# The first MLP's rank product one matmul group earlier, and the ranks behind the gating of that step

## The reference

```
attn = softmax(mask(q k^T / 8)) v            # 4 x 8 heads, 576 rows, windowed masks
h = x @ w_in;  g = h * cos(h);  y = g @ w_out                # first MLP: 2304 x 512, 2048 wide
noisy = y @ w_gate + log1p(exp(y @ w_noise)) * noise         # 8 experts
top2 of noisy; weights = softmax of the two
out[t] = sum over both choices of weight * relu(y[t] @ w1[e]) @ w2[e]   # 1024 wide
```

## Time and profile before

| | us |
|---|---|
| median of 3 runs (lowest to highest) | 1034.51 (1033.92 to 1035.71) |
| the profiled execution's own time | 1036.34 |
| its span | 1034.5 |
| TensorE busy in the span | 997.1 (96%) |
| TensorE weight loads | 877.4 (85%) |
| VectorE busy | 584.7 (57%) |
| ScalarE busy | 446.6 (43%) |
| POOL busy | 355.4 (34%) |

### The profile page before, as it was taken

How to read it: one execution, slowest core, us unless ns; L and a number is a source line. 1 busy time by engine, 2 the same in 40 slices (tenths; PEclk the granted TensorE clock), 3 DMA queues, 4 the chain that set the end, 5 groups by cost and what they waited for, 6 DMA issues and landing times. The chain is left out here.

```text
span 1034.5 us, 17745 instructions
## 1 busy us (share of the span) xinstructions
PE 997.1 (96%) x6176; PEld 877.4 (85%) x6176; DVE 584.7 (57%) x1190; ACT 446.6 (43%) x1087; POOL 355.4 (34%) x348
## 2 busy tenths in 40 slices
PE   6989899999999999999999999999999999999994
PEld 5777789888889889889887779999998889899993
DVE  4777867667576586576675744444243444444221
ACT  5878755454454544534547333333132323333110
POOL 2555687322222222222232355142341514241321
PEclk9999999999999999999999999999999999999998
DMA  8787337000000000005006154434342525333220
GB/s 171 172 183 158 76 111 266 32 2 1 30 1 0 30 1 30 1 0 183 12 11 225 59 177 133 150 99 137 139 163 106 192 109 174 126 109 108 78 69 29
DMA packets 101383, 99.63 MB, mean 96 GB/s; under 512 B 72835, under 2 KB 73315, under 8 KB 101312
## 3 DMA queue, kind: packets, MB, share of 16 engines
q1 hardware_dynamic: 89696, 67.16, 21.9%
q0 software_dynamic: 10000, 31.15, 9.6%
q10 hardware_dynamic: 1616, 0.39, 0.2%
HBM read 80.61 MB, written 20.07 MB: 97 GB/s over the span
## 5 line engine op out<-in xcount | busy, mean ns | idle before, releaser
L1740 POOL TENSOR_TENSOR g_lo<-gate,g_hi 128x384 fp32r<-128x384 f32 x95 | 98.0, 1032 | 283.4 <-ACT g_hi L1044 283.3
L1104 ACT ACTIVATE uh_hi<-ps 128x306 fp32r<-128x306 f32 (+1 forms) x112 | 47.8, 426 | 280.1 <-PE ps L155 275.0
L154 PE MATMUL ps<-ux_lo,w_hi 128*128 128x306 f32 (+1 forms) x448 | 136.5, 305 | 0.0
L155 PE MATMUL ps<-ux_hi,w_hi 128*128 128x306 f32 (+1 forms) x448 | 136.0, 304 | 0.0
L153 PE MATMUL ps<-x_hi,w_lo 128*128 128x384 f32 x384 | 134.1, 349 | 1.8 <-DVE gate L1258 1.1
L153 PE MATMUL ps<-ux_hi,w_lo 128*128 128x306 f32 (+1 forms) x448 | 135.8, 303 | 0.0
L1479 DVE SCALAR_TENSOR_TENSOR uh_lo<-ps,uh_hi 128x306 fp32r<-128x306 f32 (+1 forms) x112 | 53.3, 476 | 137.4 <-ACT uh_hi L1104 133.8
L155 PE MATMUL ps<-x_hi,w_hi 128*128 128x384 f32 x384 | 129.2, 337 | 0.0
L154 PE MATMUL ps<-x_lo,w_hi 128*128 128x384 f32 x384 | 129.2, 336 | 0.0
L153 PE MATMUL ps<-w_hi,g_lo 128*128 128x512 f32 x288 | 114.1, 396 | 0.0
L155 PE MATMUL ps<-w_hi,g_hi 128*128 128x512 f32 x288 | 114.0, 396 | 0.0
(11 more groups left out here) (225 smaller groups left out, 2002.8 us busy)
## 6 DMA issues: line engine op xcount, KB each, us to landing
xT<-in_w SPq DMA_DIRECT2D x32, 1024.0 KB, 9.1
out<-table SPq DMA_DIRECT2D x18, 256.0 KB, 3.8
y_rows<-y_sb SPq DMA_DIRECT2D x6, 768.0 KB, 3.5
y_sb<-in_w_out SPq DMA_DIRECT2D x16, 256.0 KB, 3.1
q_raw<-in_q SPq DMA_DIRECT2D x40, 96.0 KB, 2.7
v_raw<-in_v SPq DMA_DIRECT2D x28, 128.0 KB, 2.6
k_raw<-in_k SPq DMA_DIRECT2D x37, 96.0 KB, 2.9
w_raw<-in_w_in SPq DMA_DIRECT2D x4, 512.0 KB, 5.2
```

What stands on the lines that cost most here:

```text
L154: nc.tensor.matmul(psum, s_hi, m_lo, start=False, stop=False)
L155: return nc.tensor.matmul(psum, s_hi, m_hi, start=False, stop=stop)
L1104: nc.scalar.activation(u_h[0][:, f, piece_at[piece]], psH[:, f % 2, 0:PIECE[piece]], ACT.Relu).then_inc(u_hhi, 1)
L1740: nc.gpsimd.tensor_tensor(g2[1][:, f % 2, :], gate[:, f % 2, :], g2[0][:, f % 2, :], ALU.subtract).then_inc(glo_done, 1)
```

## The change

On TensorE `rank(i - 1)` (and in tile 5 `count()`) is issued at the end of step 8, behind `second(i, 6)` and ahead of `first(i, 9)`. On VectorE `route(.., 8)` is issued behind `gates(i, 8)`, ahead of `whole(i, 9)`. The one-hot rows and columns of slot products 0 and 1 stay in step 9 between `fine` and `gates`; `to_table` stays where it is, and so do `route(.., 5)` and `route(.., 6)` in step 7. No instruction is added or taken out.

```diff
@@ TensorE, tile(i)
                     first(i, f)
                     if start and f == 3:
                         second(i, 0)
-                    if not start and f == 9:
-                        rank(i - 1)
-                        if last:
-                            count()
                     if last and f >= FC - 2:
 ...
                     if last and f == FC - 1:
                         transpose_x(0)
+                    if not start and f == 8:
+                        rank(i - 1)
+                        if last:
+                            count()
                     if not start:
                         route(i - 1, f)
@@ VectorE, tile(i)
                     if not first and f == 9:
-                        route(i - 1, link, 8)
                         hots(i - 1, 0)
                     if not first and 9 <= f <= 13:
                         hots(i - 1, f - 8)
 ...
                     if not first and f == 7:
                         route(i - 1, link, 6)
+                    if not first and f == 8:
+                        route(i - 1, link, 8)
```

## The result

The changed kernel took 1039.58 us (median of 5 runs, 1039.11 to 1041.44) against 1034.51 (five runs of the kernel before by then): a ratio of 1.0049, 95% interval 1.0038 to 1.0061. The forecast was 1040.1, range 1038 to 1043.5.

A forecast was written before the change was run, and what follows sets the result against it. TensorE, busy 96% of the span, was taken to bound the kernel. Losses of 4 x 1.08 + 1.29 = 5.6 us on 1034.51 gave 1040.1, range 1038 to 1043.5 (the forecast case's own range 1038.5 to 1041.8).

The forecast's parts named there:

- The rank product: TensorE, end of step 8: it waits for the expert marks, a stall of 1.67 us in each of tiles 1 to 5.
- The terms behind it: TensorE, through first 11: a removed wait returns some 0.46 us, shorter groups 0.13; net loss 1.08 a tile, 1.29 in tile 5.
- The move on VectorE: Ranks, 1.25 us, from step 9 to step 8: costs and gives nothing on TensorE; gates(9) ends at 306.22 again.
- the hold by POOL: VectorE beside POOL's g_lo(8): one rank instruction held some 0.8 us, gates(9) ends at 307.0, still ahead of first 11.
- that rival: TensorE's clock falls after the stalls: at most 1.7 us each, 8.5 more if all five, 1048.6; chance 0.11.
- The rival without a stall: Marks are ready before TensorE reaches the moved rank product, so not slower: 1034.0 to 1034.5; chance 0.06.
- The third: Stall paid, but waits of first 10 and 11 were fixed costs: up to 1.67 us a tile, 1042.9; chance 0.08.
- The profiled execution: Whole kernel under the profiler: 1036.34 us before, forecast 1041.9; the median lies 1.83 lower, giving 1040.1.

The follow-up runs named there:

- the free product: VectorE's ranks behind gates(8), plus two bf16 matmuls on constants at the end of step 8, against the kernel before: 1034.81 us, ratio 1.0002.
- TensorE's half alone: Only the rank product (and count) moved to the end of step 8, VectorE as before, against the kernel before: 1039.98 us, ratio 1.0066.
- VectorE's half alone: Only the ranks on VectorE moved behind gates(8), rank product still in step 9, against the kernel before: 1034.67 us, ratio 1.0002.
- spread one-hots: Kernel before with one-hots of slot products 1 to 5 moved to steps 10 to 13, slot products one step behind: 1032.75 us, ratio 0.9986.
- the marks later: Changed kernel with nine copies of 8 columns ahead of the last marks instruction: 1049.25 us, ratio 1.0140 to the kernel before.

## Why the prediction was right

**The rank product.** The stall was put at 1.67 us a tile and measured 1.66. It is fixed by two times that the trace of before showed: the end of second 6 and the end of the marks. That it is the wait and not the place was argued before and is shown by the free product, and that it is the whole loss by TensorE's half alone.

**The terms behind it.** For tile 2: rank product 0.09 (forecast 0.09), first 9 2.22 (2.22), second 7 2.09 (2.08), first 10 2.08 (2.12), second 8 2.09 (2.08), two slot products 0.19 (0.14), first 11 2.15 (2.17). The loss is 1.07 (1.08). In tile 5 it is 1.23 (1.29): first 9 was 2.17 instead of 2.22 and first 11 2.12 instead of 2.17. Sum 5.49 (5.6). (Tile 1 of the kernel before was not within 0.02 us of the pattern, as the forecast had it: its first 11 took 2.18, that of tile 2 2.22.) The slot products were mis-sized, since I doubled one that follows a group, and the second costs 0.12.

**The move on VectorE** was forecast to change nothing, and VectorE's half alone gave 1.0002. The reason was partly wrong. I let whole, coarse and fine take 2.08 us in any order and bounded the hold by POOL as something added. In fact it is a trade: one of the ranks is held, and `fine(9)`, which was the one beside POOL before, is 0.62 shorter. In tiles 2, 4 and 5 it is the last of the ranks, by 0.70 us (0.87 instead of 0.17), and `gates(9)` began 4.73 us behind `gates(8)`; in tiles 1 and 3 it is the last but one, by 0.85, and they were 4.91 apart. Before, they were 4.88 apart, and the bound had allowed up to 5.7. Tile 3 of the changed kernel, where POOL's subtraction begins at 375.25:

```profile
375.25 1.02 DVE L1330 SCALAR_TENSOR_TENSOR low<-block_of,place 128x6 f32<-128x6 f32 x1
```

The Trainium skill's line in the GPSIMD Engine Reference, section Key points, on contention with instructions of two SBUF inputs fits: L1330, L1332, L1313 and L1250 all have two, and those are the ones found long beside POOL.

**The rivals.** The clock did not fall in the first MLP of the changed kernel; it did behind stalls of 2.3 us. So that rival was a real neighbour, and its chance of 0.11 was not too high. The forecast took the full clock from the page's row, where a digit stands for 26 us and a fall of 3.4 us leaves a 9 (that of 614.77 does); such a fall shows only in windows. The rival without a stall needed marks 1.6 us earlier; they came where they were expected in all five tiles. The third, with fixed costs in first 10 and 11, is refuted by the lengths above.

**The profiled execution** was forecast at 1041.9 and took 1041.44. Both profiled executions have a fall of the clock of 3.4 us in the early experts (from 614.77 and from 619.57), so it cancels in their difference.

## What to carry to other kernels

Moving a producer's consumer earlier in an in-order stream pays only if the producer is ready there. Compare two times in the trace, the end of what it waits for and the start of the slot it moves to; their difference is the cost, and everything behind it on the engine pays it, times the number of iterations. Where an engine is full between two deadlines, the order of its work changes little (where it was not full, with spread one-hots, the order cost 0.2 us a tile); taking work out of that stretch, into one where it is idle, is what moves the deadline. And before an instruction is placed next to another engine's work, look which of the neighbours is already held there: in both orders tried here the hold went to another one and did not go away.

## What the runs showed of the hardware

- Stalls of TensorE of 1.66 us left the granted clock at its full level in all five tiles of the changed kernel. Stalls of 2.31 us brought it to half (2.4 to 1.2 GHz) in three of five, with 1.5 us lost each time. The length of the idle does not decide it alone. At one place in the early experts an idle of 1.87 us in the kernel before and one of 1.88 in the changed kernel were followed by such a fall, while one of 2.02 in the kernel with TensorE's half alone and one of 2.06 in that with the marks later were not. What else decides was not tried.
- VectorE instructions with two SBUF inputs that meet POOL's subtraction of 384 columns (1.0 us) are held by it: one of 6 columns took 0.87 to 1.02 us instead of 0.17 and ended within 0.04 us of the subtraction's end, `fine` of 384 columns took 1.18 instead of 0.56. One that started 0.03 us ahead of POOL (303.16 and 303.19 in tile 2 of the changed kernel) was not held; the next one was.
- A wait that the modelled tail of the matmul before hides does not show in the list of waits: 0.4 us a tile at first 11 before, named only in the view of the weight loads. Distances between starts show it.
